# Routing index of the eight fixed expert tiles ahead of the experts, and the zero fill issued by GpSimd in the attention

## The reference

```python
def _moe_ref(x, w_skip, w_gate, w1, w2):
    skip_score = x @ w_skip
    do_compute = skip_score > 0
    out = x.copy()
    xc = x[do_compute]
    logits = xc @ w_gate
    e_idx = np.argmax(logits, axis=1)
    logits_s = logits - logits.max(-1, keepdims=True)
    probs = np.exp(logits_s)
    probs /= probs.sum(-1, keepdims=True) + 1e-09
    gate_w = probs[np.arange(len(xc)), e_idx]
    y = np.zeros_like(xc)
    for e in range(8):
        mask = e_idx == e
        y[mask] = gate_w[mask, None] * (np.maximum(xc[mask] @ w1[e], 0.0) @ w2[e])
    out[do_compute] = xc + y
    return out

def reference(**inputs):
    # attention: 4 batches, 8 heads, 576 positions, head size 64;
    # heads 0-3 see the last 32 positions, heads 4-7 every 32nd one
    attn = softmax(mask(q @ k.T / 8)) @ v
    x = attn.transpose(0, 2, 1, 3).reshape(2304, 512)
    x = _moe_ref(x, w_skip, w_gate, w1, w2)     # 8 experts, 512 -> 1024 -> 512
    h = x @ w_in                                # 512 -> 2048
    return np.maximum(0.01 * h, h) @ w_out      # 2048 -> 512
```

## Time and profile before

| | |
|---|---|
| median of the runs | 772.04 us (771.41, 772.04, 774.05) |
| the profiled execution | 777.4 us |
| its span, first to last instruction | 775.2 us |
| mean granted TensorE clock | 0.974 of full speed |
| busy: PE, DVE, ACT, POOL | 716.9, 276.2, 262.0, 180.5 us |
| DMA: from SP's and POOL's queues | 66.14 MB and 24.79 MB |

### The profile page before, as it was taken

How to read it: one execution, slowest core, us unless ns; L and a number is a source line. 1 busy time by engine, 2 the same in 40 slices (tenths; PEclk the granted TensorE clock), 3 DMA queues, 4 the chain that set the end, 5 groups by cost and what they waited for, 6 DMA issues and landing times.

```text
span 775.2 us, 12846 instructions
## 1 busy us (share of the span) xinstructions
PE 716.9 (92%) x4628; PEld 664.1 (86%) x4628; DVE 276.2 (36%) x578; ACT 262.0 (34%) x522; POOL 180.5 (23%) x182
## 2 busy tenths in 40 slices
PE   2989979993699999998999999999999999999997
PEld 2878868873699999997999999998989899999986
DVE  4667656757100000003332333233333333332222
ACT  4687666651111112212222223322232322222222
POOL 2120100011686666562100310040031004001000
PEclk9999998986699999999999999999999999999999
DMA  8483746779799999972100210030012004001001
GB/s 175 107 188 100 168 102 171 218 236 229 168 317 341 300 314 338 315 248 64 43 1 0 70 54 1 7 116 1 1 59 63 0 0 122 0 0 41 1 0 41
DMA packets 73112, 91.46 MB, mean 118 GB/s; under 512 B 26704, under 2 KB 47728, under 8 KB 73073
## 3 DMA queue, kind: packets, MB, share of 16 engines
q1 hardware_dynamic: 63969, 66.14, 29.7%
q0 software_dynamic: 8048, 24.79, 11.3%
q10 hardware_dynamic: 1056, 0.02, 0.1%
HBM read 73.91 MB, written 17.01 MB: 117 GB/s over the span
## 4 chain that ended last, share of the span: by engine, by line
PE 74%; SPq 10%; DMA 5%; DVE 3%; issue 3%; ACT 2%; another core or an unknown queue 2%; ACTq 0%; DVEq 0%; POOLq 0%
PE psum L1584 26%; PE psum L1603 26%; PE psum L1497 8%; PE psum L1513 8%; SPq L401 6%; DMA x_rows<-xo 3%; SPq L396 2%; SPq L386 1%; ACT kt L797 1%; PE psum L1336 1%; PE psum L1523 1%; PE psum L1566 1%; DMA x_sb<-x_rows 1%; SPq L409 1%
## 5 line engine op out<-in xcount | busy, mean ns | idle before, releaser
L1584 PE MATMUL psum<-x2h,wih 128*128 128x384 f32 x384 | 130.6, 340 | 1.9 <-DVE x2l L1256 1.9
L1274 DVE SCALAR_TENSOR_TENSOR g_act<-g_raw 128x384 f32<-128x384 f32 x96 | 53.6, 558 | 219.4 <-ACT g_raw L960 205.9
L1584 PE MATMUL psum<-x2h,wil 128*128 128x384 f32 x384 | 129.5, 337 | 0.0
L1584 PE MATMUL psum<-x2l,wih 128*128 128x384 f32 x384 | 129.0, 336 | 0.0
L960 ACT ACTIVATE g_raw<-psum 128x384 f32<-128x384 f32 x96 | 47.2, 492 | 235.3 <-PE psum L1584 232.0
L1603 PE MATMUL psum<-woh,g_l 128*128 128x512 f32 x288 | 114.0, 396 | 0.0
L1603 PE MATMUL psum<-wol,g_h 128*128 128x512 f32 x288 | 113.7, 395 | 0.0
L1603 PE MATMUL psum<-woh,g_h 128*128 128x512 f32 x288 | 112.1, 389 | 0.7 <-DVE g_l L1278 0.7
L1497 PE MATMUL psum<-xt,wring 128*128 128x160 f32 x512 | 80.9, 305 | 0.6 <-issue 0.6
L759 POOL DMA_INDIRECT out_dram<-o_sb,idxo x15 | 15.9, 1061 | 277.8 <-ACT o_sb L955 274.8
L1513 PE MATMUL psum<-hp,wring 128*128 128x160 f32 x512 | 77.6, 299 | 0.0
(11 more groups left out here) (177 smaller groups left out, 899.2 us busy)
## 6 DMA issues: line engine op xcount, KB each, us to landing
wring<-in_moe_w_dram SPq DMA_DIRECT2D x64, 512.0 KB, 8.6
y_rows<-zrow SPq DMA_DIRECT2D x1, 4800.0 KB
q_st<-in_q_dram SPq DMA_DIRECT2D x8, 576.0 KB
k_st<-in_k_dram SPq DMA_DIRECT2D x8, 576.0 KB
x_sb<-x_rows SPq DMA_DIRECT2D x4, 1024.0 KB, 6.4
stage<-in_moe_w_in_dram POOLq DMA_DIRECT2D x4, 1024.0 KB, 9.0
stage<-in_moe_w_out_dram POOLq DMA_DIRECT2D x4, 1024.0 KB, 9.2
vs<-in_v_dram SPq DMA_DIRECT2D x20, 128.0 KB, 7.6
```

The source lines that it names most:

```text
L1274: dve.scalar_tensor_tensor(out=g_act[:, f % 2, :], in0=g_raw[:, f % 2, :], scalar=LEAK, in1=g_raw[:, f % 2, :], op0=ALU.mult, op1=ALU.max) ...
L1584: last = pe.matmul(bank[f % 2][:, 0:MT * P], wt[:, c, f * P:(f + 1) * P], xp[:, T.par, c, :], start=(c == 0 and n == 0), stop=(c == KD - 1 ...
```

## The change

1. POOL issues the zero fill, in three pieces, each behind its copy of q in the attention's loop (`zero_rows`), from 100 partitions of `zrow` with each row sent 8 times. SP's fill is gone; those who waited for it wait for `s_zf` too.
2. `LOG` comes from a matmul with `comb` (two identities one above the other) in place of a transpose, so that PE adds the two halves; DVE's copy and addition are gone, and the one-hot is made in fewer steps.
3. The slots of the eight fixed tiles (16 halves) are worked out first, from the rank alone. Only their one-hots (`eq_b`, `row_b`, `tok_b`) are made ahead of the first gather, without POOL.
4. Plan, general slots, the one-hots of the 28 overflow halves, the gate's weights and the positions come after it on DVE. PE makes the overflow index in the first tile at f == 5 (`TIDX_O`), and DVE finishes it there (`overflow_index`, `s_tok_o`). POOL waits for it ahead of its first `stage_split`. ACT makes both halves of the first `x_copy`.

```diff
-    ZC = 20
+    ZC = 24
     FILL = (SKIP - (E - 1) * TILE) // ZC
...
+    HB, HO = 2 * E, NHALF - 2 * E
...
-        TIDX = bank[4][0:HALF, 0:2 * NHALF]
+        TIDX = bank[4][0:HALF, 0:2 * HB]
+        TIDX_O = bank[2][0:HALF, 0:2 * HO]
...
             sp.dma_start(y_d[SKIP:SKIP + 1, :], zrow[0:1, :]).then_inc(s_zd, 16)
-            sp.dma_start(y_d[(E - 1) * TILE:SKIP, :].rearrange("(p c) n -> p c n", p=FILL),
-                         zrow[:, :].unsqueeze(1).to_broadcast([FILL, ZC, D])).then_inc(s_zd, 16)
...
+            step(pool.tensor_tensor(comb[:, :], ident[0:LW, 0:E + 1], ident[0:LW, E + 1:LW], ALU.add))
...
+            def zero_rows(b):
+                c0 = b * (ZC // (B - 1))
+                part = y_d[(E - 1) * TILE:SKIP, :].rearrange("(p c) n -> p c n", p=FILL)
...
+                pool.dma_start(part, zrow[:, :].unsqueeze(1).to_broadcast(
+                    [FILL, ZC // (B - 1), D])).then_inc(s_zf, 16)
...
                     pool.tensor_copy(to, what).then_inc(s_in, 1)
+                    if dst is q_in:
+                        zero_rows(b)
...
-            for part in range(2):
-                t_ = slice(part * NR, part * NR + NR)
-                pool.wait_ge(s_r, R_HALVES + 2 * part)
-                pool.tensor_tensor(oh_tok[:, t_, 1, :], eq_half[:, t_, :],
-                                   c_t[:, t_].unsqueeze(2).to_broadcast([P, NR, NHALF]),
-                                   ALU.mult).then_inc(s_hott, 1)
...
+                if i == 0:
+                    pool.wait_ge(s_tok_o, 1)
                 stage_split(i)
...
             x_copy(0, 0)
+            act.wait_ge(s_xt, 2)
+            act.activation(xt[:, 0, :, HALF:TILE],
+                           bank[3][:, 0:KD * HALF].rearrange("d (c t) -> d c t", c=KD),
+                           ACT.Copy).then_inc(s_xf[1], 1)
...
-            step(dve.tensor_copy(ls[:, :, :], LOG[:, :, 0:E + 1]))
-            step(dve.tensor_tensor(ls[:, :, :], LOG[:, :, E + 1:LW], ls[:, :, :], ALU.add))
...
+            step(dve.reduce_max(lmax[:, :], LOG[:, :, 0:E], AX.X))
+            dve.tensor_tensor(sh[:, :, :], LOG[:, :, 0:E], free(lmax[:, :], T3, 2), ALU.subtract
+                              ).then_inc(s_sh, 1)
+            dve.wait_ge(s_sh, 1)
+            step(dve.scalar_tensor_tensor(out=eqp[:, :, :], in0=sh[:, :, :], scalar=0.0,
+                                          in1=free(c_pref[:, :], T3, 1), op0=ALU.is_ge, op1=ALU.mult))
+            dve.tensor_scalar(ohb[:, 0:NT, 0], skips, 0.0, None, ALU.is_le).then_inc(s_one, 1)
+            step(dve.reduce_max(kmax[:, :], eqp[:, :, :], AX.X))
+            step(dve.scalar_tensor_tensor(out=kskip[:, :], in0=skips, scalar=0.0, in1=kmax[:, :],
+                                          op0=ALU.is_le, op1=ALU.add))
+            dve.tensor_tensor(ohb[:, 0:NT, 1:E + 1], eqp[:, :, :], free(kskip[:, :], T3, 2), ALU.is_equal
+                              ).then_inc(s_one, 1)
...
             dve.wait_ge(s_rk, 1)
+            step(dve.tensor_tensor(posn[:, :, :], RANK[:, 0:NT, :], ohb[:, 0:NT, 1:E + 1], ALU.mult))
+            step(dve.reduce_sum(rank[:, :], posn[:, :, :], AX.X))
...
+            dve.tensor_tensor(eq_b[:, :, :], free(hid0[:, :], HB3, 2), free(c_half[:, 0:HB], HB3, 1),
+                              ALU.is_equal).then_inc(s_eqb, 1)
+            dve.tensor_tensor(row_b[:, 0:NR, :], free(row0[:, 0:NR], R3, 2), free(c_row[:, :], R3, 1),
+                              ALU.is_equal).then_inc(s_rowb, 1)
+            dve.wait_ge(s_eqb, 1)
+            dve.tensor_tensor(tok_b[:, :, 1, :], eq_b[:, :, :], free(c_t[:, :], HB3, 2), ALU.mult
+                              ).then_inc(s_tokt, 1)
+            dve.tensor_tensor(row_b[:, NR:NT, :], free(row0[:, NR:NT], R3, 2), free(c_row[:, :], R3, 1),
+                              ALU.is_equal).then_inc(s_rowb, 1)
...
+            dve.wait_ge(s_ti, 1)
+            step(dve.tensor_copy(tok_t[:, 0:HB], TIDX[:, 0:HB]))
+            dve.scalar_tensor_tensor(out=tok_idx[:, 0:HB], in0=TIDX[:, HB:2 * HB], scalar=float(P),
+                                     in1=tok_t[:, 0:HB], op0=ALU.mult, op1=ALU.add).then_inc(s_plan, 1)
...
+            def overflow_index():
+                dve.wait_ge(s_ti_o, 1)
+                step(dve.tensor_copy(tok_t[:, HB:NHALF], TIDX_O[:, 0:HO]))
+                dve.scalar_tensor_tensor(out=tok_idx[:, HB:NHALF], in0=TIDX_O[:, HO:2 * HO],
+                                         scalar=float(P), in1=tok_t[:, HB:NHALF], op0=ALU.mult,
+                                         op1=ALU.add).then_inc(s_tok_o, 1)
...
-                        last = pe.transpose(LOG[:, 2 * j + u, :], lt[:, j % 2, u * P:(u + 1) * P],
-                                            ident[0:LW, 0:LW])
+                        last = pe.matmul(LOG[:, 2 * j + u, :], lt[:, j % 2, u * P:(u + 1) * P],
+                                         comb[:, :], start=True, stop=True)
...
+                    if first and f == 5:
+                        for hf in range(2):
+                            pe.wait_ge(s_xf[hf], 2)
+                        pe.wait_ge(s_hot_o, 3)
+                        for t in range(NT):
+                            last = pe.matmul(TIDX_O, row_o[:, t, :],
+                                             tok_o[:, t, :, :].rearrange("p a h -> p (a h)"),
+                                             start=(t == 0), stop=(t == NT - 1))
+                        last.then_inc(s_ti_o, 1)
```

More of the change, by code:

```diff
@@ L94, in attention_experts_mlp @@
     wg = at(keep, "wg", [P, KD, E + 1])
+    comb = at(keep, "comb", [2 * (E + 1), E + 1])
     wgs = at(keep, "wgs", [P, KD, 2 * (E + 1)], F32R)
-    ZC = 20
+    ZC = 24
     FILL = (SKIP - (E - 1) * TILE) // ZC
@@ L247, in attention_experts_mlp @@
         s_r = sem("s_r")
+        s_sh = sem("s_sh")
+        s_one = sem("s_one")
+        s_eqb = sem("s_eqb")
+        s_rowb = sem("s_rowb")
+        s_tokt = sem("s_tokt")
+        s_hot_o = sem("s_hot_o")
+        s_ti_o = sem("s_ti_o")
+        s_tok_o = sem("s_tok_o")
         s_rex = sem("s_rex")
@@ L873, in _ @@
                     act.activation(lt[:, i % 2, :], LGT[i % 2], ACT.Copy).then_inc(s_lt, 1)
-            act.wait_ge(s_r, R_SHIFTED)
+            act.wait_ge(s_sh, 1)
             act.activation(ex[:, :, :], sh[:, :, :], ACT.Exp).then_inc(s_rex, 1)
[L877 to L881, removed]
+            act.wait_ge(s_eqb, 1)
+            act.activation(tok_b[:, :, 0, :], eq_b[:, :, :], ACT.Copy, scale=c_p[:, 0:1]).then_inc(s_hot, 1)
             def x_copy(j, par):
@@ L1120, in _ @@
-            step(dve.tensor_scalar(esum[:, :], esum[:, :], 1e-9, None, ALU.add))
-            step(dve.reciprocal(esum[:, :], esum[:, :]))
-            step(dve.tensor_tensor(rec[:, :, 2].bitcast(F32), esum[:, :], takes[:, :], ALU.mult))
-            dve.wait_ge(s_rk, 1)
+            dve.wait_ge(s_rk, 1)
+            step(dve.tensor_tensor(posn[:, :, :], RANK[:, 0:NT, :], ohb[:, 0:NT, 1:E + 1], ALU.mult))
+            step(dve.reduce_sum(rank[:, :], posn[:, :, :], AX.X))
+            dve.scalar_tensor_tensor(out=h80[:, :], in0=rank[:, :], scalar=float(HALF), in1=half2[:, :],
+                                     op0=ALU.is_ge, op1=ALU.add).then_inc(s_r, 1)
@@ new lines, in _ @@
+            dve.tensor_scalar(far[:, :], rank[:, :], float(TILE), 1000.0, ALU.is_ge, ALU.mult
+                              ).then_inc(s_r, 1)
+            dve.tensor_scalar(r80[:, :], rank[:, :], float(HALF), -float(HALF), ALU.is_ge, ALU.mult
+                              ).then_inc(s_r, 1)
+            n_[0] += 3
+            dve.wait_ge(s_r, n_[0])
+            dve.tensor_tensor(hid0[:, :], h80[:, :], far[:, :], ALU.add).then_inc(s_r, 1)
+            n_[0] += 1
+            step(dve.tensor_tensor(row0[:, :], rank[:, :], r80[:, :], ALU.add))
@@ new lines, in _ @@
+            dve.tensor_tensor(tok_o[:, :, 1, :], eq_o[:, :, :], free(c_t[:, :], HO3, 2), ALU.mult
+                              ).then_inc(s_hot_o, 1)
+            step(dve.tensor_copy(rec[:, :, 1], slot[:, :]))
+            dve.wait_ge(s_rex, 1)
+            step(dve.reduce_sum(esum[:, :], ex[:, :, :], AX.X))
+            step(dve.tensor_scalar(esum[:, :], esum[:, :], 1e-9, None, ALU.add))
+            step(dve.reciprocal(esum[:, :], esum[:, :]))
+            step(dve.tensor_tensor(rec[:, :, 2].bitcast(F32), esum[:, :], takes[:, :], ALU.mult))
@@ L1466, in _ @@
                 if t % NR == 0:
-                    pe.wait_ge(s_r, R_HOTS if t else R_HOTS0)
-                    pe.wait_ge(s_hot, 2 if t else 1)
-                    pe.wait_ge(s_hott, 2 if t else 1)
-                last = pe.matmul(TIDX, oh_row[:, t, :],
-                                 oh_tok[:, t, :, :].rearrange("p a h -> p (a h)"), start=(t == 0),
-                                 stop=(t == NT - 1))
+                    pe.wait_ge(s_rowb, t // NR + 1)
+                    pe.wait_ge(s_hot, 1)
+                    pe.wait_ge(s_tokt, 1)
```

(4 more changed lines are left out.)

132 lines of the change are left out of this document (65 added, 67 removed).

## The result

The changed kernel takes **788.24 us** (median of 787.67 to 789.61, four runs) against 771.81 us for the kernel before, run beside it (771.41 to 774.05): a ratio of 1.0209, with an interval of 1.0185 to 1.0234. That is slower by about 16 us, where 768.6 was predicted and 774.0 was the end of the range.

The account below looks back on a forecast made before the run. PE was taken to bound the experts, a chain of waits the router. The terms -1.15 + 0.7 - 0.4 - 4.3 - 0.8 + 0.85 + 1.7 = -3.4 took 772.04 to 768.6 us, range 765.6 to 774.0.

Parts of the forecast that it names:

- the work fits, but it meets the loads: Attention: three fill pieces fit into idle DMA time but delay loads; plus 1.7 us (0.5, 0.2, 1.0), bounds 0 and 7.
- Rival (b): Attention: 100-row pieces run on ten engines and stretch SP's issues; 8 us lost, slower at 774.9; chance 0.12.
- rival (a): Attention: the fill costs there what the router gains, 3 to 7 us lost, time 770 to 774; chance 0.22.
- -5.1 of the rest: Whole kernel: the sum of all terms without the fill's cost in the attention, -5.1 us.
- Front of the router: First DVE router step to PE: fewer steps cut 3.18 us to 2.03, minus 1.15.
- Clock of the rank matmuls: Router: PE, called back 1.1 us sooner, may begin the 19 rank matmuls at 2.4 GHz; minus 0.4 us.
- Ranks to index: Router, from ranks to token index: fewer one-hots and no Pool multiplication cut 9.56 us to 5.3, minus 4.3.
- Index to the first expert matmul: First gather: with the fill gone it lands in 3.9 us in place of 5.33; minus 0.8, bounds minus 0.2 and 1.5.
- Overflow index: First expert tile: eighteen added matmuls on a PE that is never idle; plus 0.85 us, bounds 0.7 and 1.4.
- `comb` and the router's matmuls: Router's front: true f32 matmuls replace transposes, three and a half pairs on the chain; plus 0.7 us, bounds 0 and 1.0.
- Rival (c): Experts: the second gather there lands late, PE waits 2.3 us at the third x_turn, time 770.9; chance 0.10.
- Rival (d): Router: the index isn't much sooner, or the new matmuls cost double; time 770; chance 0.05.

Follow-up runs that it names:

- e3: The kernel before with only the zero fill changed, to three pieces issued by Pool in the attention: 790.49 us, ratio 1.0211.
- e2: The changed kernel with the fill's pieces sent from 80 rows, 10 times each, in place of 100 rows 8 times: 779.81 us, ratio 1.0081.
- e1: The changed kernel with the zero fill back on SP as one DMA of 120 rows, no piece in the attention: 774.24 us, ratio 0.9999.
- e5: e4 with the second half of the first expert's weights moved behind the gathers, so the fill starts right behind the x loads: 767.89 us, ratio 0.9931.
- e4: e1 without `comb`: PE transposes `lt`, DVE copies and adds the halves; 773.39 us, ratio 0.9999.
- e8: e1 with Pool's gather of the third tile ahead of its wait for the overflow index and the first split: 771.64 us, ratio 0.997.
- e10: e5 with Pool's third tile gather ahead of its overflow index wait and first split, fill on 120 rows: 767.42 us, ratio 0.9925.
- e6: e5 with Pool's third tile gather moved earlier and the fill sent by SP from 80 rows: 768.07 us, ratio 0.9917.

## Why the prediction was wrong

**The step that failed** is "the work fits, but it meets the loads", with "plus 1.7" as the fill's price and "0 and plus 7" as its bounds. In the profiles the attention ends 15.8 us later. By the medians it is more: they are 16.4 us apart, and everything behind the attention became 4.0 us shorter, which makes 20.4. The ends of the attention in the kernels without a fill there (150.3 to 155.6, against 171.9) give 16 to 22. e3 shows that it is the fill alone: 2.1% on a kernel without the rest. All else that was predicted is worth a few microseconds beside it. Two things were wrong in the step.

First, capacity was counted where occupancy counts. A mean share of 0.60 says that bytes fit in; it doesn't say what happens to the queue of small loads behind them. The earlier trace rows held the answer: an issue on SP goes from 0.78 to 1.72 where engines are backed up. I applied that to parts of one or two pieces. It holds for most of each piece: 2.18, 1.82, 2.15 and 1.95 us in a row, 5.1 us lost in the first one.

Second, nearly all of it reached the end, as all three pieces lie where SP is on the chain. The delay between the two profiles was 4.0 us after the first piece, 9.8 at the third copy of q, and 15.8 at the end of the attention: 4 to 6 for each piece, and none of them was made up again.

**Rival (b)** was right in both mechanisms, ten engines and stretched issues, and in the sign. It was given 0.12 and a price of 8 us. Its 6 us for a piece that meets SP's chain fully is about what was measured (4.0, 5.8 and 6.0 between the two profiles). What it had wrong is that it let the three pieces meet the chain only in part: three times 6 is 18, and that lies within the 16 to 20 measured. Its two other numbers, 12.3 us for a piece (13.6 measured) and 1.72 for an issue (about 2.0), are smaller errors; and 12.3 doesn't come out of its own rows, as 215 GB/s at a share of 0.92 give 11.2 us on ten engines. The ten engines are only half of it. With 16 of them (e2) 1.3 of the 2.1% are gone, some 10 us. What is left of the fill's price is the 0.8%, some 6 us, by which e2 is slower than before, and the 4 us that became shorter behind the attention: about 10 us. So rival (a), with 3 to 7 us, was too low as well.

**What the prediction didn't see** is that the -5.1 of the rest and the fill hang together. The router gains that only while no fill is in its way. With the fill on SP (e1), the way from the index to the first expert matmul takes 5.9 us longer than in after, and next to nothing is left of the gain. Moved into the attention, the fill costs 16 to 20. e5 shows the third way: it starts earlier in SP's order, beside the router's matmuls, and 0.7% are gained.

The other terms, from the two profiles:

- Front of the router: -1.15 predicted, 3.18 to 2.02 us measured.
- Clock of the rank matmuls: -0.4 predicted, nothing came. 1.76 us from their start to DVE's next step against 1.75: the clock was at its low level (0.54 in the window from 198 to 202), though PE had stood still for only 2.13 us, in place of 3.29. In e4 it was still high after 2.86 us, and 18 of them took 0.84. So the length of this wait alone didn't decide it. The bounds, 0 and -0.6, hold both.
- Ranks to index: -4.3 predicted, 9.56 to 5.15 measured, so -4.4.
- Index to the first expert matmul: -0.8 predicted, -1.7 measured; the gather landed in 2.93, under the 3.9 that I took. The first three groups of the first tile then took 6.42 us in place of 5.38, as the clock stayed low for longer (still 0.56 from 217 to 219, over 4 us after the first of them, where before has 1.00 from 206 on, 4 us after it); no term had that.
- Overflow index: +0.85 predicted, 0.68 measured.
- `comb` and the router's matmuls: +0.7 predicted; from the end of the last `xo` to the first DVE step 24.8 in place of 22.6 us. The term took three and a half pairs of token tiles to be on the chain. PE bounds the whole loop, so that each turn counts, with 0.31 us. The low clock at the start isn't the difference: the first 16 transposes take 3.68 us in after and 3.67 in before.
- Rival (c), the late third gather: nothing in after, 1.0 us of idle PE in e1; moving it earlier was worth 2 us by e8 and nothing by e10. The margin of 0.4 was as thin as said.
- Rival (d) fell: the index came as soon as predicted.
- The low end of the range, 765.6, isn't the sum of the three bounds that the prediction names for it; they give 766.0.

The sum of the profiles: 15.8 (attention), 2.3 (matmuls of the router), -5.6 (first step to index), -1.7 (index to experts) and 1.0 (the rest, with the overflow index and the longer low clock in it) make 11.8.

## What to carry to other kernels

Before bulk traffic is moved into idle DMA time, ask who is on the chain there: where a queue of many small loads is, each of its issues may take nearly three times as long for most of the time that the bulk is under way (0.75 to about 2.0 us here), and the mean busy share doesn't show that. Choose the number of rows of a large DMA so that 16 divides it: 80 rows in place of 100 won back 1.3% here. (Between 120 and 80 rows, in e10 and e6, no difference showed.) Count a term in full where its engine bounds the whole loop, as PE did with `comb`. And when a consumer is made earlier, look at what was hidden in the time that goes: here the gather ran into the fill, and it took starting the fill earlier for the faster router to show in the time.

## What the runs showed of the hardware beyond that

- A piece of 1.64 MB sent out of 100 or 50 rows lands in 13.6 or 14.1 us, and out of 80 rows in 9.7 (medians of three pieces), with 60% and 96% of the 16 engines' time taken by the piece.
- The issue of a v load (31.5 KB) by SP takes 0.75 us with little beside it and mostly 1.5 to 2.3 us beside a piece that Pool issued, with 80 rows as with 100, though the two have queues of their own.
- An indirect DMA of 80 rows of 2 KB, one of two in a row, lands in 2.9 to 3.1 us with no fill beside it, and in 9.65 to 9.98 in the middle of a fill of 4.9 MB from another queue.
